# A linear-attention and two-MLP kernel: attention units of two head pairs by two chunks in six equal stages

## The chip, the cores and the metric

The kernel runs on one core of a Trainium2 chip. The metric is the device time of one execution in microseconds. The kernel before took 366.56 us (median of 3 runs, 365.85 to 368.96).

## What is computed

The reference, cut to what matters (batch 2, 8 heads, 768 steps, head size 48, model size 384, hidden size 1024, all float32):

```python
for t in range(S):                      # attention with a decaying state
    cur = np.einsum('bhd,bhe->bhde', u[None] * kt, vt)
    y[:, :, t] = np.einsum('bhd,bhde->bhe', rt, state + cur)
    state = wt[:, :, :, None] * state + np.einsum('bhd,bhe->bhde', kt, vt)
...
xk = mu_k * x + (1.0 - mu_k) * x_prev   # first MLP, x_prev is x one step back
xr = mu_r * x + (1.0 - mu_r) * x_prev
k = np.maximum(xk @ w_k, 0.0)
v = k * k @ w_v
r = 1.0 / (1.0 + np.exp(-(xr @ w_r)))
x = r * v
...
h = gelu(x @ w_in)                      # second MLP, u and v are h's halves
v_s = np.einsum('ts,bsd->btd', w_sg, layernorm(v)) + b_sg[None, :, None]
out = x + (u * v_s) @ w_out
```

## The kernel before

The 12 chunks of 128 steps (6 in each batch) are grouped into five **stages** of 2, 2, 2, 3 and 3 chunks (`CHUNKS`). In a stage there are four attention **units**, one for each pair of heads (`PAIRS`); a head takes 64 of the 128 partitions (`SLOT`), 48 of them used. There are 20 units. A unit passes over the engines in three steps:

- VectorE, `scan` and `scale_keys` (L987 to L1026): running products of the decays w (`prod`), r times k (`rkp`), reciprocals of the ends, `r_in`, the products from the back (`suffix`), and the scaled keys `k_in`.
- TensorE, `first` (L592): coefficients r·k·u into `pkt`, transposes of `k_in`, and the scores into `ps`. ScalarE copies coefficients and transposed keys (`coef`, `k_tok`) and writes the diagonal tiles of `att` (L860), one 128x128 instruction for each chunk and head. VectorE overwrites the part above the diagonal with the scores (`mask`, L1033). TensorE, `second` (L618): keys times values into `pu`. VectorE adds the state (`carry_on`, tile `z`) and ScalarE multiplies it by the decay (L879, tiles `inner` and `carry`).
- TensorE, `third` (L635): state times `r_in` and `att` times values into `py`. ScalarE copies `py` to `y_sb`; SyncE moves it into `X`, from head rows to model rows, with two or three small transfers a unit (`segments`, `give_output`, L463).

Once all four units of a stage are in `X`, ScalarE and VectorE mix it with itself one step back (`xf`) and split it into a high and a low float32r part (`xkr_h`, `xkr_l`). TensorE then computes the **first MLP** of the stage with three matmuls for each product (`three`, L332 to L334: high·high, high·low, low·high): 27 matmuls for r, 72 for k and 72 for v, each as wide as the stage has steps (256 or 384). They are cut into tiles of at most 512 columns in three PSUM banks. ScalarE and VectorE split the squared relu of each k tile again (`k2_h`, `k2_l`, in the trace `k_h`, `k_l`), and v's matmuls wait for it.

The order is set by slots: in slot `i` each engine works unit `i` (VectorE's scan), unit `i - 1` (`first`, `mask`, `second`) and unit `i - 2` (`third`), and the pieces of the first MLP that `PIECES` puts there, from slot `FIRST_MLP` = 7 on. Weights are split into high and low parts in fixed slots (`WSPLIT`). A second, plain form of the attention exists for decays far from 1: ScalarE checks all of w ahead, in four pieces (`flat_w`, L776 and L778), TensorE sums the counts, and at slot `CHOICE` VectorE and SyncE load the flag and branch over the plain form.

SyncE issues every load: `wb` (decays by stage), `rk` and `vb` (by unit), `flat_w`, and the weights.

The **second MLP** (`ORDER2`, 686 of the 2389 matmul records) follows when all stages are done, over all eight PSUM banks.

## Time and profile before

| | |
|---|---|
| median of 3 runs | 366.56 us |
| the profiled execution | 368.12 us, of which the span is 366.4 us |
| TensorE matmuls busy | 333.6 us, 91% of the span |
| VectorE busy | 220.3 us, 60% |
| ScalarE busy | 180.6 us, 49% |
| GpSimd busy | 43.4 us, 12% |
| DMA | 28.98 MB |

The profile is of one execution. Busy time of TensorE is the union of overlapping matmuls with modelled ends. In a timeline "us" is the length of one instruction or of a run of like ones, while the rate is read from one start to the next. A number in brackets is the idle time of the engine just before the instruction, with what ended it. A float32 matmul shows as two records, so "x8" of scores are four matmuls; a float32r matmul (L332 to L334) is one.

### The profile page before, as it was taken

To read this page: it belongs to the slowest core of one execution; us is meant where nothing else is said; L and a number is where in the kernel's file an instruction comes from. 1 tells how busy PE (TensorE), PEld (TensorE's weight loads), DVE (VectorE), ACT (ScalarE), POOL (GpSimd) and SP (SyncE) were. 2 spreads that over 40 slices of the span, in tenths; PEclk is the share of its full clock that TensorE was granted. 3 is DMA by queue.
4 is the path that set the end of the run, shared out by engine and by line. 5 is a ranking of instruction groups with operands and counts; after the bars stand their busy time and mean duration, and the time that the engine had idled before them with its cause. 6 is when DMAs were issued, how large, how long until landed. Compare 5 with 4: busy or idle time off the path is not lost.

```text
span 366.4 us, 6535 instructions
## 1 busy us (share of the span) xinstructions
PE 333.6 (91%) x2389; PEld 311.6 (85%) x2389; DVE 220.3 (60%) x417; ACT 180.6 (49%) x404; POOL 43.4 (12%) x54
## 2 busy tenths in 40 slices
PE   3876649969999899979999999999999999999996
PEld 2654439968899789968999999989999998999996
DVE  5567672896489866788448548369363445503332
ACT  1899565673457565756558457256511303521110
POOL 2000000000000000000000000027423303803320
PEclk9999958989999989998999999999999999999999
DMA  7997114202540242110000601520000030000012
GB/s 212 401 362 231 55 53 143 56 5 69 174 136 13 83 118 62 51 40 16 18 16 2 226 7 24 237 86 0 2 0 2 0 108 23 1 2 0 2 43 86
DMA packets 15632, 28.98 MB, mean 79 GB/s; under 512 B 2160, under 2 KB 10224, under 8 KB 15600
## 3 DMA queue, kind: packets, MB, share of 16 engines
q1 hardware_dynamic: 15600, 28.56, 23.7%
q8 instruction: 19, 0.31, 0.4%
q14 instruction: 13, 0.11, 0.1%
HBM read 23.83 MB, written 2.36 MB: 71 GB/s over the span
## 4 chain that ended last, share of the span: by engine, by line
PE 69%; DVE 13%; ACT 9%; issue 7%; DMA 1%; DVEq 1%; SPq 0%; ACTq 0%
PE pm L332 14%; PE pm L334 13%; PE pm L333 13%; PE ps L334 3%; PE ps L333 3%; PE ps L332 3%; DVE att L1033 2%; ACT att L860 2%; PE py L649 2%; PE ps L614 2%; PE py L655 2%; DVE suffix L1014 2%; DVE prod L996 1%; DVE xf L1076 1%; PE pkt L334 1%
## 5 line engine op out<-in xcount | busy, mean ns | idle before, releaser
L332 PE MATMUL pm<-k_h,wv_h 128*128 128x256 f32 (+1 forms) x120 | 38.4, 320 | 2.8 <-issue 2.8
L556 POOL TENSOR_TENSOR rstd<-vare,half_neg 128x1 f32<-128x1 f32 x12 | 9.4, 784 | 261.0 <-DVE vare L1186 261.0
L334 PE MATMUL pm<-k_h,wv_l 128*128 128x256 f32 (+1 forms) x120 | 37.5, 313 | 0.0
L333 PE MATMUL pm<-k_l,wv_h 128*128 128x256 f32 (+1 forms) x120 | 37.5, 312 | 0.0
L332 PE MATMUL pm<-xkr_h,wk_h 128*128 128x256 f32 (+1 forms) x120 | 37.3, 311 | 0.0
L334 PE MATMUL pm<-xkr_h,wk_l 128*128 128x256 f32 (+1 forms) x120 | 36.4, 304 | 0.0
L333 PE MATMUL pm<-xkr_l,wk_h 128*128 128x256 f32 (+1 forms) x120 | 36.4, 303 | 0.0
L1100 DVE TENSOR_TENSOR sq<-relu 128x384 f32<-128x384 f32 (+1 forms) x28 | 17.2, 614 | 28.6 <-ACT relu L813 28.4
L860 ACT ACTIVATE att<-ident,coef 128x128 f32<-128x128 f32 x96 | 30.3, 394 | 0.0
L935 ACT CAST gated_h<-gf 128x384 fp32r<-128x384 f32 x16 | 8.2, 514 | 42.9 <-DVE gf L1208 42.9
L879 ACT ACTIVATE inner<-z,prod 128x128 f32<-128x128 f32 x28 | 11.2, 402 | 34.1 <-DVE z L1053 22.1
L332 PEld LDWEIGHTS pm<-k_h,wv_h 128*128 128x128 f32 x120 | 24.0, 200 | 4.2 <-issue 4.2
L614 PE MATMUL ps<-r_in,k_in 48*128 48x128 f32 x192 | 19.7, 339 | 8.0 <-DVE att L1033 8.0
L614 PEld LDWEIGHTS ps<-r_in,k_in 48*128 48x128 f32 x192 | 15.3, 226 | 12.8 <-issue 12.8
L813 ACT ACTIVATE relu<-pm 128x384 f32<-128x384 f32 (+1 forms) x28 | 14.9, 533 | 18.8 <-PE pm L334 18.6
L333 PEld LDWEIGHTS pm<-k_l,wv_h 128*128 128x128 f32 x120 | 24.1, 200 | 0.0
L334 PEld LDWEIGHTS pm<-k_h,wv_l 128*128 128x128 f32 x120 | 23.9, 199 | 0.0
L332 PEld LDWEIGHTS pm<-xkr_h,wk_h 128*128 128x128 f32 x120 | 22.8, 190 | 1.0 <-issue 0.7
L333 PEld LDWEIGHTS pm<-xkr_l,wk_h 128*128 128x128 f32 x120 | 22.8, 190 | 0.0
L334 PEld LDWEIGHTS pm<-xkr_h,wk_l 128*128 128x128 f32 x120 | 22.8, 190 | 0.0
L601 PE MATMUL pkt<-par,rkp 128*128 128x2 f32 x96 | 16.0, 277 | 6.4 <-DVE rkp L1001 6.4
L583 POOL TENSOR_TENSOR gated_l<-gf,gated_h 128x384 fp32r<-128x384 f32 x16 | 16.2, 1011 | 46.7 <-ACT gated_h L935 36.5
(227 smaller groups left out, 915.3 us busy)
## 6 DMA issues: line engine op xcount, KB each, us to landing
rk<-in_rkT SPq DMA_DIRECT2D x12, 256.0 KB, 3.8
rk<-in_rkT SPq DMA_DIRECT2D x8, 384.0 KB, 3.4
flat_w<-in_w SPq DMA_DIRECT2D x4, 576.0 KB, 9.5
wsg_raw<-in_wsgT SPq DMA_DIRECT2D x1, 2304.0 KB, 10.4
out_y<-y_out SPq DMA_DIRECT2D x12, 192.0 KB, 1.9
wb<-in_wT SPq DMA_DIRECT2D x2, 776.0 KB, 4.8
vb<-in_vT SPq DMA_DIRECT2D x12, 128.0 KB, 3.6
wk_raw<-in_moe_w_k SPq DMA_DIRECT2D x3, 512.0 KB, 11.2
```

The source lines that it names most:

```text
L332: pe.matmul(o, a_h, b_h, start=first and n == 0, stop=False)
L333: pe.matmul(o, a_h, b_l, start=False, stop=False)
L334: mm = pe.matmul(o, a_l, b_h, start=False, stop=last and n == len(pairs) - 1)
L556: pool.tensor_tensor(rstd[:, t:t + 1], vare[:, t:t + 1], half_neg[:], ALU.pow).then_inc(rstd_done, 1)
L583: pool.tensor_tensor(gated_l[:, x, cols], gf[:, ng % 2], gated_h[:, x, cols], ALU.subtract).then_inc(gl_done, 1)
L601: pe.matmul(pkt[:, MAXT + 2 * ch:MAXT + 2 * ch + 2], rkp[:, p, ch * C:(ch + 1) * C], u_col[:, g], start=True, stop=True)
L614: mm = pe.matmul(ps[:, h, cols], k_in[head, p, cols], r_in[head, un % 3, cols], start=True, stop=True)
L813: act.activation(relu[:, j % 2, 0:G * T], o, ACT.Relu).then_inc(m_free[bk], 1)
L860: last = act.activation(att[:, b % 2, h, ch * C:(ch + 1) * C], ident[:], ACT.Identity, scale=coef[:, b % 2, 2 * ch + h:2 * ch + h + 1])
L879: act.activation(to, z[:, zi % NZ], ACT.Identity, scale=prod[:, b % 2, ch, C:C + 1]).then_inc(state_done, 1)
L935: act.copy(gated_h[:, x, cols], gf[:, ng % 2]).then_inc(gh_done, 1)
L1100: dve.tensor_tensor(sq[:, j % 2, both], relu[:, j % 2, both], relu[:, j % 2, both], ALU.mult).then_inc(sq_done, 1)
```

## The change

- All stages have two chunks (`N` = 2), so there are six, each with two units; a unit holds two head pairs by two chunks, four blocks of 128 steps (`BLOCKS`). There are 12 units. In stage `s`, the loops below call the next stage's units `a` = 2s + 2 and `b` = 2s + 3.
- The inputs of a unit (decays, r, k) come in one load of 790 KB (`load_unit`); for unit 0 it is split, the decays on SyncE's queue and r and k on ScalarE's, which also loads the parameters.
- Coefficients go to the end of `pu`, beside the key-value products, so `first` waits for the state steps of the unit before (`z_done`). The state keeps 64 columns for a head pair; TensorE reads only the 48 rows of a head. VectorE does all state steps, four 128x128 ones for both pairs of a unit, and ScalarE none.
- The check of w is done by unit, on the loaded decays, and the choice is made for each stage; the plain form, if chosen, runs for that stage.
- All first-MLP tiles are 256 wide. The orders of SyncE, TensorE, ScalarE and VectorE are written out, with loops over the stages.
- `mixed`, `gf` and `vf` of the second MLP have other places in memory. The second MLP's instructions and their order are the same.

```diff
-CHUNKS = ((0, 0, 2), (0, 2, 2), (0, 4, 2), (1, 0, 3), (1, 3, 3))
-LONGEST = 3
 PAIRS = 4
+N = 2
+T = N * C
+BLOCKS = 2 * N
+WIDE = BLOCKS * C
+W1 = BLOCKS * (C + 1) + 1
+UNIT = W1 + 2 * WIDE
...
+            def load_unit(un):
+                if un == 0:
+                    sp.dma_start(inw[:, 0, 0:W1], units[:, 0:W1]).then_inc(s_in[0], 16)
+                    return
+                if un >= 3:
+                    sp.wait_ge(kin_done, un - 2)
+                    sp.wait_ge(rkp_done, un - 2)
+                    sp.wait_ge(checked, un - 2)
+                sp.dma_start(inw[:, un % 3], units[:, un * UNIT:(un + 1) * UNIT]).then_inc(s_in[un % 3], 16)
...
+            def give_output(un):
+                s, q, _, _ = place(un)
+                sp.wait_ge(y_done, un + 1)
+                for pr in range(2):
+                    for row, kt, f, m in segments(2 * q + pr):
+                        sp.dma_start(X[f:f + m, s % 2, kt, 1:T + 1],
+                                     y_sb[row:row + m, un % 2, pr * T:(pr + 1) * T]).then_inc(x_in[q], 16)
...
+            load_unit(0)
+            load_unit(1)
+            load_v(0)
+            load_part(0)
+            load_v(1)
+            load_part(1)
+            load_part(2)
+            load_unit(2)
+            load_part(3)
+            load_v(2)
+            for j in parts_of("wv"):
+                load_part(j)
+            give_output(0)
+            give_output(1)
+            choose(0)
+            for s in range(STAGES - 1):
+                for un in (2 * s + 3, 2 * s + 4):
+                    if un < NU:
+                        load_unit(un)
+                        load_v(un)
+                give_output(2 * s + 2)
+                give_output(2 * s + 3)
+                choose(s + 1)
...
                 if un:
                     pe.wait_ge(coef_done, un)
+                    pe.wait_ge(z_done, z_count(un))
+                for m in range(BLOCKS):
+                    mm = pe.matmul(pu[:, COEF + 2 * m:COEF + 2 * m + 2], rkp[:, p, m * C:(m + 1) * C],
+                                   u_col[:, 2 * q + m // N], start=True, stop=True)
+                if q == 1:
+                    pe.wait_ge(checked, un + 1)
+                    mm = pe.matmul(pu[0:1, FLAG:FLAG + un + 1], ones[:], outside[:, 0:un + 1], start=True, stop=True)
+                mm.then_inc(c_mm, 1)
+                pe.wait_ge(kin_done, un + 1)
+                if un:
...
+                pe.wait_ge(inner_done, un + 1)
+                if c0:
+                    pe.wait_ge(carry_done, carry_count(un - 1))
...
+                pe.wait_ge(att_done, un + 1)
...
-            for i in range(SLOTS):
-                b, c = unit(i, 1), unit(i, 2)
-                before, after = parts(i)
-                if b is not None:
+            first(0)
+            second(0)
+            first(1)
+            second(1)
+            third(0)
+            third(1)
+            for s in range(STAGES):
+                a, b = 2 * s + 2, 2 * s + 3
+                if 0 < s < STAGES - 1:
+                    first(a)
+                    second(a)
+                for tile in RS + KS[:1]:
+                    first_mlp(s, *tile)
+                if s == 0:
+                    first(a)
+                    second(a)
+                    for tile in KS[1:]:
+                        first_mlp(s, *tile)
+                    third(a)
                     first(b)
-                if c is not None:
-                    third(c)
-                for tile in before:
-                    first_mlp(*tile)
-                if b is not None:
                     second(b)
-                for tile in after:
-                    first_mlp(*tile)
-                if i == CHOICE:
-                    pe.wait_ge(outside_done, NCHK)
-                    pe.matmul(pm[0][0:1, 0:NCHK], ones[:, 0:1], outside[:], start=True, stop=True).then_inc(flag_sum, 1)
+                    first_mlp(s, *VS[0])
+                    third(b)
+                    first_mlp(s, *VS[1])
+                else:
+                    if s < STAGES - 1:
+                        third(a)
+                        first(b)
+                        second(b)
+                    for tile in KS[1:]:
+                        first_mlp(s, *tile)
+                    if s < STAGES - 1:
+                        third(b)
+                    for tile in VS:
+                        first_mlp(s, *tile)
...
+            act.dma_start(inw[:, 0, W1:UNIT], units[:, W1:UNIT]).then_inc(s_first, 16)
+            act.dma_start(par[:], params).then_inc(s_par, 16)
...
-            def check(n):
-                act.activation(q, q, ACT.Square, bias=minus_one[:, 0:1]).then_inc(sq_w, 1)
...
+                decays = inw[:, un % 3, 0:W1 - 1].rearrange("p (m t) -> p m t", m=BLOCKS)[:, :, 1:C + 1]
+                act.activation(junk[:], decays, ACT.Square, bias=minus_one[:, 0:1]).then_inc(sq_w, 1)
+                act.wait_ge(sq_w, un + 1)
+                act.activation(junk[:], junk[:], ACT.Relu, bias=minus_one[:, 0:1], scale=RANGE ** -2,
+                               accum_out=outside[:, un:un + 1]).then_inc(checked, 1)
...
-                        to = inner[:, b % 2, ch] if ch < n - 1 else carry[:, g, s % 2]
-                        act.activation(to, z[:, zi % NZ], ACT.Identity,
-                                       scale=prod[:, b % 2, ch, C:C + 1]).then_inc(state_done, 1)
...
+            check(0)
+            act.wait_ge(s_par, 16)
+            coefs(0)
+            keys(0)
+            diagonals(0)
+            check(1)
+            coefs(1)
+            diagonals(1)
+            keys(1)
+            high_weight(0)
+            high_weight(1)
+            output(0)
+            high_weight(2)
+            output(1)
+            high_weight(3)
+            mix(0)
+            for s in range(STAGES):
+                a, b = 2 * s + 2, 2 * s + 3
+                more = s < STAGES - 1
+                if s and more:
+                    coefs(a)
+                    keys(a)
+                    diagonals(a)
+                if more:
+                    check(a)
+                gate(s, *RS[0])
+                gate(s, *RS[1])
+                key_high(s, 0)
+                if more:
+                    check(b)
+                if s == 0:
+                    coefs(a)
+                    keys(a)
+                    diagonals(a)
+                    for n in range(1, KG):
+                        key_high(s, n)
+                        high_weight(parts_of("wv")[n - 1])
+                    high_weight(parts_of("wv")[KG - 1])
+                    output(a)
+                    coefs(b)
+                    keys(b)
+                    diagonals(b)
+                    output(b)
+                    mix(s + 1)
+                elif more:
+                    output(a)
+                    coefs(b)
+                    keys(b)
+                    diagonals(b)
+                    for n in range(1, KG):
+                        key_high(s, n)
+                    output(b)
+                    mix(s + 1)
+                else:
+                    for n in range(1, KG):
+                        high_weight(parts_of("win")[n - 1])
+                        key_high(s, n)
                     split_x2(0)
...
+                added = pu[:, 0:COEF].rearrange("p (r c e) -> p r c e", r=2, c=N)
+
+                def total(ch):
+                    return prod[:, p, ch:BLOCKS:N, C:C + 1].to_broadcast([P, 2, SLOT])
+
                 dve.wait_ge(u_mm, un + 1)
+                if un:
+                    dve.wait_ge(inner_done, un)
+                if c0:
+                    dve.wait_ge(carry_done, carry_count(un - 1))
+                    dve.tensor_tensor(z[:, 0], added[:, :, 0], carry[:, (s - 1) % 2, q], ALU.add).then_inc(z_done, 1)
+                else:
+                    dve.tensor_copy(z[:, 0], added[:, :, 0]).then_inc(z_done, 1)
+                dve.wait_ge(z_done, z_count(un) + 1)
+                if un >= 2:
+                    dve.wait_ge(y_mm, un - 1)
+                dve.tensor_tensor(inner[:, p], z[:, 0], total(0), ALU.mult).then_inc(inner_done, 1)
+                if len(steps(un)) == N:
+                    dve.wait_ge(inner_done, un + 1)
+                    if carry_count(un):
+                        dve.wait_ge(carry_done, carry_count(un))
+                    dve.tensor_tensor(z[:, 1], added[:, :, 1], inner[:, p], ALU.add).then_inc(z_done, 1)
+                    dve.wait_ge(z_done, z_count(un + 1))
+                    dve.tensor_tensor(carry[:, s % 2, q], z[:, 1], total(1), ALU.mult).then_inc(carry_done, 1)
...
+                mix_now(s, 0)
+                mix_now(s, 1)
+                mix_low(s, 0)
+                mix_now(s, 2)
+                mix_low(s, 1)
+                mix_low(s, 2)
...
+            scan(0)
+            scan_back(0)
+            dve.wait_ge(s_par, 16)
+            dve.tensor_scalar(omu[:], mu, -1.0, 1.0, ALU.mult, ALU.add).then_inc(omu_done, 1)
+            scan(1)
+            scan_back(1)
+            mask(0)
+            carry_on(0)
+            mask(1)
+            carry_on(1)
+            low_weight(0)
+            scan(2)
+            choose(0)
+            dve.wait_ge(omu_done, 1)
+            mix(0)
+            for j in parts_of("wk"):
+                low_weight(j)
+            scan_back(2)
+            for s in range(STAGES):
+                a, b = 2 * s + 2, 2 * s + 3
+                if s == 0:
+                    key_low(s, 0)
+                    mask(a)
+                    carry_on(a)
+                    key_low(s, 1)
+                    scan(b)
+                    key_low(s, 2)
+                    scan_back(b)
+                    key_low(s, 3)
+                    for j in parts_of("wv"):
+                        low_weight(j)
                     mask(b)
                     carry_on(b)
-                for tile in after:
-                    first_mlp(*tile)
-                for j in range(len(WSPLIT)):
-                    if WSPLIT[j][4] == i:
-                        low_weight(j)
-                if i == END + 2:
-                    split_x2(0)
-                if i == CHOICE:
-                    choose()
+                    scan(b + 1)
+                    scan_back(b + 1)
+                    choose(s + 1)
+                    mix(s + 1)
+                elif s < STAGES - 1:
+                    mask(a)
+                    carry_on(a)
+                    scan(b)
+                    scan_back(b)
+                    key_low(s, 0)
+                    mask(b)
+                    carry_on(b)
+                    key_low(s, 1)
+                    if b + 1 < NU:
+                        scan(b + 1)
+                    key_low(s, 2)
+                    if b + 1 < NU:
+                        scan_back(b + 1)
+                    key_low(s, 3)
+                    choose(s + 1)
+                    mix(s + 1)
+                else:
+                    key_low(s, 0)
+                    for n in range(1, KG):
+                        low_weight(parts_of("win")[n - 1])
+                        key_low(s, n)
+                    for kt in range(KT):
+                        split_x2(0, kt)
+                for tile in VS:
+                    value(s, *tile)
```

TensorE at the start of the program. Before, units follow one another with `third` (L649, L655) of unit 0 after `first` (L601, L605, L614) of unit 1:

```order
L601 MATMUL pkt<-par,rkp 128x2 x2
L605 MATMUL pkt<-ident,k_in 128x128 x2
L614 MATMUL ps<-r_in,k_in 128x128 x4
L629 MATMUL pu<-vb,k_tok 64x64 x4
L601 MATMUL pkt<-par,rkp 128x2 x2
L605 MATMUL pkt<-ident,k_in 128x128 x2
L614 MATMUL ps<-r_in,k_in 128x128 x4
L649 MATMUL py<-r_in,inner 64x128 x2
L655 MATMUL py<-att,vb 64x128 x4
L629 MATMUL pu<-vb,k_tok 64x64 x4
L601 MATMUL pkt<-par,rkp 128x2 x2
L605 MATMUL pkt<-ident,k_in 128x128 x2
```

All of six such units pass before the first L332. After, with four blocks a unit, from the transposes of unit 0 on (L540, L544, L550 and L559 are `first`, L576 `second`, L598 and L605 `third`):

```order
L550 MATMUL pkt<-ident,k_in 128x128 x4
L559 MATMUL ps<-r_in,k_in 128x128 x8
L576 MATMUL pu<-vb,k_tok 64x64 x8
L540 MATMUL pu<-par,rkp 128x2 x4
L544 MATMUL pu<-outside,ones 1x2
L550 MATMUL pkt<-ident,k_in 128x128 x4
L559 MATMUL ps<-r_in,k_in 128x128 x8
L576 MATMUL pu<-vb,k_tok 64x64 x8
L598 MATMUL py<-r_in,inner 64x128 x4
L605 MATMUL py<-att,vb 64x128 x8
L598 MATMUL py<-r_in,inner 64x128 x4
L605 MATMUL py<-att,vb 64x128 x8
```

The row after the last one is the first matmul of the first MLP. Both `third` have moved behind both `second`, and two units stand before the MLP where six stood.

VectorE in the middle of the program. Before, between the mix of stage 1 and that of its third tile (L1086 is `xkr_l`, L1114 the product with v, L1033 `mask`, L1053 the state, L996 to L1023 the scans):

```order
L1086 TENSOR_TENSOR xkr_l<-xf,xkr_h 128x2x256 x2
L1114 TENSOR_TENSOR x_116<-pm,x_116 128x2x256
L1033 COPY_PREDICATED att<-upper,ps 128x2x256
L1053 TENSOR_TENSOR z<-pu,carry 128x128
L1076 SCALAR_TENSOR_TENSOR xf<-X,omu,xf 128x256 x2
L996 SCALAR_TENSOR_TENSOR prod<-wb,one 128x258
L1001 TENSOR_TENSOR rkp<-rk 128x256
L1005 RECIPROCAL ends<-prod 128x2
L1008 TENSOR_TENSOR r_in<-rk,prod 128x256
L1014 SCALAR_TENSOR_TENSOR suffix<-wb,ends 128x258
L1023 TENSOR_TENSOR k_in<-rk,suffix 128x256
L1086 TENSOR_TENSOR xkr_l<-xf,xkr_h 128x2x256
```

After, between the mix of stage 3 and the first k tile (L1077, L1114, L1030 and L1048 to L1061 are the same steps):

```order
L1114 TENSOR_TENSOR x_116<-pm,x_116 128x256
L1030 COPY_PREDICATED att<-upper,ps 128x1024
L1048 TENSOR_TENSOR z<-pu,carry 128x128
L1054 TENSOR_TENSOR inner<-z,prod 128x128
L1059 TENSOR_TENSOR z<-pu,inner 128x128
L1061 TENSOR_TENSOR carry<-z,prod 128x128
L997 SCALAR_TENSOR_TENSOR prod<-inw,one 128x516
L1003 TENSOR_TENSOR rkp<-inw 128x512
L1007 RECIPROCAL ends<-prod 128x4
L1010 TENSOR_TENSOR r_in<-inw,prod 128x512
L1018 SCALAR_TENSOR_TENSOR suffix<-inw,ends 128x516
L1023 TENSOR_TENSOR k_in<-inw,suffix 128x512
```

The four state operations now stand in a row on VectorE, each waiting for the one before. The scans of the stage's second unit have moved behind mask and states of its first unit, and the whole mix of a stage stands in one piece ahead of them.

## Rows read from the trace of the kernel before

**Rows 1.** Windows by stage of the first MLP: us, busy us of each engine, PEclk.

```profile
core 0: us, PE busy (x) PEld busy (x) DVE busy (x) ACT busy (x) POOL busy (x), PEclk, DMA share, GB/s
0.00:54.50 54.50, 32.59 (x228) 25.37 (x228) 36.32 (x83) 35.99 (x85) 1.92 (x14) 0.91 0.64 218
54.50:93.70 39.20, 35.74 (x318) 32.93 (x316) 26.92 (x57) 23.46 (x58) 0.00 (x0) 0.91 0.26 75
93.70:132.00 38.30, 36.18 (x355) 33.23 (x353) 29.76 (x59) 22.67 (x63) 0.00 (x0) 0.97 0.33 105
...
209.20:238.80 29.60, 29.60 (x172) 29.60 (x172) 16.45 (x25) 14.89 (x25) 0.00 (x0) 1.00 0.29 103
238.80:366.40 127.60, 124.67 (x686) 120.12 (x684) 58.38 (x103) 37.12 (x66) 41.44 (x40) 1.00 0.08 25
```

**Rows 2.** Timeline of TensorE, 256-wide matmuls: start, us, instruction.

```profile
94.13 0.28 PE L332 MATMUL pm<-xkr_h,wr_h 128*128 128x256 f32 x1
...
94.49 0.28 PE L332 MATMUL pm<-xkr_h,wr_h 128*128 128x256 f32 x1
```

**Rows 3.** Timeline of TensorE, attention between MLP matmuls, two and three chunks.

```profile
99.62 0.50 PE L601 MATMUL pkt<-par,rkp 128*128 128x2 f32 x4
...
102.00 0.39 PE L332 MATMUL pm<-xkr_h,wk_h 128*128 128x256 f32 x1
...
181.64 0.72 PE L601 MATMUL pkt<-par,rkp 128*128 128x2 f32 x6
...
185.01 0.44 PE L332 MATMUL pm<-xkr_h,wk_h 128*128 128x384 f32 x1
```

**Rows 4.** Timeline of VectorE: front halves of a two-chunk and a three-chunk unit, masks.

```profile
92.61 0.70 DVE L996 TENSOR_TENSOR_SCAN prod<-wb,one 128x258 f32<-128x258 f32 x1 [0.58 <-ACT inner L879]
...
95.00 0.74 DVE L1033 COPY_PREDICATED att<-upper,ps 128x512 f32<-128x512 uint32 x1
...
122.76 0.96 DVE L996 TENSOR_TENSOR_SCAN prod<-wb,one 128x387 f32<-128x387 f32 x1
...
126.08 0.69 DVE L1086 TENSOR_TENSOR xkr_l<-xf,xkr_h 128x512 fp32r<-128x512 f32 x1
...
127.02 1.00 DVE L1033 COPY_PREDICATED att<-upper,ps 128x768 f32<-128x768 uint32 x1
```

**Rows 5.** The page: GB/s moved in 40 equal slices of 9.16 us.

```profile
GB/s 212 401 362 231 55 53 143 56 5 69 174 136 13 83 118 62 51 40 16 18 16 2 226 7 24 237 86 0 2 0 2 0 108 23 1 2 0 2 43 86
```

**Rows 6.** Timeline of TensorE: the same score matmuls early and late.

```profile
37.92 1.23 PE L614 MATMUL ps<-r_in,k_in 48*128 48x128 f32 x8
...
62.81 0.72 PE L614 MATMUL ps<-r_in,k_in 48*128 48x128 f32 x8
```

**Rows 7.** Timelines of ScalarE and SyncE, the chain, DMA issues (us to landing).

```profile
114.43 1.86 ACT L860 ACTIVATE att<-ident,coef 128x128 f32<-128x128 f32 x6
...
23.53 1.80 SPq L463 DMA_DIRECT2D X<-y_sb  x3
...
X<-y_sb SPq DMA_DIRECT2D x22, 48.0 KB, 2.0
...
40.93 0.54 DVEq L979
```

**Rows 8.** Groups by form: engine, operation, count, busy us, mean ns, idle before.

```profile
L1076 DVE SCALAR_TENSOR_TENSOR xf<-X,omu,xf 128x256 f32<-128x256 f32 x18 | 7.7, 481 | 2.7 <-ACT xf L790 2.5
L1086 DVE TENSOR_TENSOR xkr_l<-xf,xkr_h 128x512 fp32r<-128x512 f32 x9 | 5.9, 686 | 0.7 <-ACT xkr_h L799 0.7
L1120 DVE TENSOR_TENSOR wv_l<-wv_raw,wv_h 128x768 fp32r<-128x768 f32 x4 | 3.6, 951 | 0.0
L1100 DVE TENSOR_TENSOR sq<-relu 128x512 f32<-128x512 f32 x12 | 8.3, 690 | 14.7 <-ACT relu L813 14.7
L778 ACT ACTIVATE flat_w<-flat_w,minus_one 128x1152 f32<-128x1152 f32 x4 | 5.0, 1255 | 0.1
```

**Rows 9.** Timeline of TensorE at a wait, and the window around it.

```profile
161.97 0.94 PE L614 MATMUL ps<-r_in,k_in 48*128 48x128 f32 x12 [2.11 <-DVE att L1033]
...
159.00:170.00 11.00, 8.82 (x82) 7.91 (x82) 9.52 (x17) 5.18 (x14) 0.00 (x0) 0.84 0.16 45
```

880 lines of the change are left out of this document (347 added, 533 removed).

## The prediction

> **What bounds the kernel now.** I began with the busy shares on the page: TensorE 91% of the span, VectorE 60%, ScalarE 49%. The reader should see there that TensorE looks like the bound, and distrust it, since its ends are modelled and an average hides stages. So next comes the table by stage [rows 1], cut where the first MLP's matmuls of each stage begin. The span falls into three parts. From 0 to 54.5 the first MLP has not started; TensorE is busy 32.6 of 54.5 us with small matmuls. From 54.5 to 238.8 the five stages run; the first two take 39.2 and 38.3 us, the last 29.6. From 238.8 to 366.4 the second MLP runs, 127.6 us, at full clock and busy nearly throughout. The diff leaves the third part's instructions and their order alone, so I take it as unchanged and forecast only when it starts.
>
> Matmul rates come from start to start, not from the "us" column: a 256-wide matmul follows the one before it after 0.12 us (0.36 for three) [rows 2], a 384-wide one after 0.173 (171 of them fill the last stage, 29.6 us) [rows 1]. An attention unit of two chunks takes 2.38 us from its coefficients to the end of its outputs, one of three chunks 3.37 [rows 3].
>
> **The matmul work.** Before, the first MLP is 3 stages of 171 at 0.12 and 2 of 171 at 0.173: 61.3 + 59.3 = 120.6 us. After, it is 6 x 171 x 0.12 = 122.6, so 2 us more. Per column a narrow matmul is dearer than its width: 256 columns at 2.4 GHz are 0.107 us and 384 are 0.16, both 0.013 below the rows. The Trainium skill ("TensorE: Matmul & The Clock Gate", section "Wait — 56ns, not 53.3ns?") puts the fixed part at about 2.5 ns for one matmul; by it the sixth stage's 171 extra matmuls would cost 0.4 us. By the rows they cost 2, and I use the rows. Attention: four blocks, extrapolated from 2.38 and 3.37, take 4.4, and their key-value products about 0.6: 5.0 us a unit, 10 a stage. A full stage is then 20.4 + 10.0 + 0.5 of changeovers = 31 us of TensorE. The work is the same as before; the term that can change is what TensorE waits for.
>
> **The start.** Before, four units of stage 0 (and two more) have to pass before any MLP. After, two fat units do. Chain, in us from the span's start. VectorE works a unit's front half (products, reciprocals, r_in, suffix, k_in) in 2.39 for two chunks and 3.32 for three [rows 4], so 4.25 for four blocks. The data of unit 0 are 0.8 MB: at 212 GB/s in the first slice [rows 5] 3.7 us after issues near 1, and a first latency near 1: in at about 5.8, and its keys ready at 9.4. TensorE is slow here: eight score matmuls' records take 1.23 us at 37.9 and 0.72 at 62.8 [rows 6], while the granted clock is given as 0.91 on average [rows 1]; the two durations are those of its two levels, 1.2 and 2.4 GHz, so I price its work until the MLP at 1.7 times. Transposes 1.2, key copy 0.6, eight diagonals at 0.295 (1.86 for six [rows 7]) end at 13.9; the mask (0.74 for 512, 1.00 for 768 elements [rows 4], so 1.27 for 1024) and two state steps end at 16.1. `first(1)` now waits for those (z_done, a new wait: behind it on TensorE stand unit 1's coefficients, transposes and scores and both `third`, and ScalarE's `coefs(1)` waits for them), then 1.3 + 1.2 + 2.3 and `second(1)` 1.3: 22.4. `third(0)` and `third(1)` at 3.0 each: 28.4. Output copy 0.6. Then SyncE issues five X transfers a unit at 0.6 each (1.80 for three [rows 7]); the last lands 2.0 after its issue [rows 7]: 33.6. The mix of stage 0 (two 0.48 steps, a cast and a 0.69 subtraction for each of three kt [rows 8], ScalarE in between) takes 4.7 after that. First MLP matmul at 38 instead of 54.5: **16 us early**.
>
> Unit 0's second half comes on ScalarE's queue. The Trainium skill ("Trainium Kernel Development and Optimization", section "Key Constraints") says that transfers issued from SP and ACT share the same 16 DMA engines and interleave, so the extra queue saves issue time only. By it unit 1's 790 KB share the engines with unit 0's 524 KB; the 5.8 above would be 6.5 and the start 0.7 later. No run here shows two queues.
>
> **Stage 0** gives much of that back. First stage: slow clock over its first 3.4 us (1.7 lost, as at 54.5); `second(2)` waits for the keys behind ScalarE's checks (1.1); `first(3)` waits for VectorE's suffix scan behind two key subtractions (2.3); the v tiles wait for the four wv subtractions (0.95 each [rows 8]), which VectorE reaches after `key_low(0, 3)` (2.5). Worst is the end: `third(3)` stands between the two v tiles, so its output, 4.5 us of transfers and 4.7 of mixing have 2.9 us of v matmuls and 2.5 of `first(4)` as cover. That leaves TensorE waiting 5 to 7 us, and the r matmuls of stage 1 start at about 85. Stage 0 lasts 46.5 us against 39.2: **7.3 lost**.
>
> **Stages 1 to 4.** VectorE's work in one: two front halves 8.5, masks 2.5, states 3.0 (eight operations of about 0.28 and a hand-over), four key pairs 5.6 (2 x 0.69 each [rows 8]), mix 4.4, v products 1.0, `choose` 1.1 (its load of the flag 0.54 [rows 7] and the branch): 26. Below 31, but it is not free to slide. The chain from the end of one stage's v tiles: coefficients and transposes 1.4, keys 0.65, diagonals 2.45, mask 1.3, states 1.5, front half of b 4.35: 11.65. `key_low(0)` 1.4, then a wait for b's diagonals until 15.4, mask and states 18.2, key pair 19.6, scan 22.05, key pair 23.45, suffix 25.35, last key pair 26.75. TensorE stands at the last quarter of v's first sum at 24.65 and so waits 2.1 us; 6.45 us of v matmuls follow. Period **33.2**, against 31 for TensorE alone. A wait of 2.1 us is in the trace once [rows 9], and TensorE's clock is low after it (0.84 in 159 to 170); 3.3 us of matmuls at half rate cost 1.65. I count that in about half of the stages. Stage 1 is 1.5 shorter (last chunks have no second state). Stage 4 has no scans ahead and no wait, so 31; its mix ends 1 us late.
>
> Sum: r matmuls of stage 1 at 85; v ends 31.7, 33.2, 33.2 and 30.5 later counted from 82.5, which gives 211; mix wait 1.4; last stage 20.4 and 1.2 behind the w_in subtractions: 234. Half of four slow spells would add 3, and against it I take off 2 for handovers counted twice: the second MLP starts at **235 instead of 238.8**. Span 362.6, with the 1.7 around it 364.3 against the profiled 368.1. The runs' median is 366.56, so I forecast 366.6 - 4 = **362.5**.
>
> **Bounds of what no row shows.** A four-block step lies between the three-chunk row and twice the two-chunk row: front half 3.3 to 4.8, mask 1.0 to 1.5, attention unit 3.4 to 4.8; I take the continued line from two to three. A state step with a broadcast factor lies between 0.28 and 0.35 and a hand-over of 0.1 comes on top. `choose` costs VectorE 0.5 to 1.1. Each of these at its upper end lengthens a stage's chain by 1 to 1.5 us, at its lower end shortens it by the whole 2.1.
>
> **Edits that I price at nothing.** The check of w moves from four 1152-wide pairs on ScalarE to twelve 512-wide ones (10 us becomes about 15) and 2.3 MB of loads go. One 1152-wide step is 1.25 [rows 8]; by width and a fixed part a 512-wide one is about 0.65. ScalarE is at 23 busy of 38 in a stage [rows 1]. If the cover fails (a check stands before `coefs(a)` in stage 0) it is 1.4 each, 5 in all. State decays leave ScalarE (40 operations) for 22 small ones on VectorE, in the chain above. X transfers: 50 before, 60 after, since each stage has ten. On SyncE's queue they now stand behind the next two units' loads, whose waits (`kin_done`, `y_mm` of the stage before) are over by then, so nothing is added; were one of them late, X and with it the mix would be late by the same. The 48 state rows for 128 change no column count; between nothing and 0.1 us a unit.
>
> **Rivals.**
> (B) VectorE keeps up. If b's diagonals come earlier or the state steps are shorter, the waits disappear and so do the slow spells: 3 x 2.1, 1.4 and 1.2 less than 234, and the same 2 off: second MLP at 223, 16 earlier, time **351**. For it: VectorE has 26 of 31. Against: the chain crosses four engines and I found no slack in it.
> (C) The other side. The chain is the bound in every stage and grows with hand-overs of 0.1 to 0.2 that I left out. It decides from a period of 35.5 on: 2.3 more in four stages and 1.65 of slow clock in two more, 235 + 9.2 + 3.3 = 247.5, which is 8.7 after 238.8: **375**. For it: before, the stages lose 4 to 7 us to such waits already, and their loose order (one unit behind) gives more slack than the new one.
> (D) The start is not early. Two-chunk units of two pairs double every latency of the chain; if unit 0's data land at 8 and the X transfers queue behind the wv loads, the MLP starts at 43, five later than forecast: second MLP at 240, time **368**. For it: half of the chain is slow TensorE. Against: 6.9 MB are in by 22 us at the rates of the first slices (212, 401 and 362 GB/s) [rows 5], before X is needed.
>
> **How the numbers follow.** Forecast 0.45 (its own range 358 to 367), B 0.22, C 0.20, D 0.13. A measurement here can tell about 1%, 3.7 us. Faster than 362.9: 0.6 of the forecast's share and B's, 0.48. Within 1%: 0.31. Slower: most of C and a little of D, 0.21. The range leaves out the far halves of B and C: 353 to 374.
>
> **What would show it.** Right: first MLP matmul near 38; its wait for v tiles and X around 70 to 84; stages 1 to 3 of 33 to 35 us; a 2 us wait of TensorE on k_l in the first v tile of each, with a fall of its clock after; the second MLP starting near 235 and lasting 127.6. Wrong: stage periods of 31 (B) or over 35.5 (C), a start after 42 (D), or a second MLP whose length differs, which I have no reason for.

## The result, and the profile after

The changed kernel takes 369.6 us (median of 6 runs, 368.3 to 371.1) against 366.8 (6 runs of the kernel before): ratio 1.008, 95% interval 1.004 to 1.011. That is within 1%, on the slow side. The forecast was 362.5, faster.

The profiled execution took 370.85 us, with a span of 369.1. These are the windows of the changed kernel, cut where each stage's first MLP matmuls begin, so that they answer to [rows 1]:

```profile
core 0: us, PE busy (x) PEld busy (x) DVE busy (x) ACT busy (x) POOL busy (x), PEclk, DMA share, GB/s
0.00:38.50 38.50, 18.14 (x139) 15.17 (x139) 21.62 (x39) 20.56 (x46) 2.15 (x14) 1.00 0.62 224
38.50:88.10 49.60, 41.37 (x361) 38.72 (x361) 32.05 (x50) 24.66 (x58) 0.00 (x0) 0.87 0.18 62
88.10:122.40 34.30, 33.36 (x320) 31.44 (x317) 23.41 (x40) 20.81 (x51) 0.00 (x0) 0.94 0.25 83
122.40:157.00 34.60, 32.45 (x313) 30.51 (x309) 24.11 (x42) 20.24 (x50) 0.00 (x0) 0.95 0.22 74
157.00:190.00 33.00, 31.62 (x322) 29.69 (x318) 24.02 (x42) 20.19 (x50) 0.00 (x0) 1.00 0.15 45
190.00:219.30 29.30, 28.38 (x275) 26.82 (x274) 18.03 (x31) 18.67 (x45) 0.00 (x0) 1.00 0.16 45
219.30:241.50 22.20, 20.72 (x171) 20.55 (x172) 12.86 (x17) 12.07 (x17) 0.00 (x0) 1.00 0.41 157
241.50:369.10 127.60, 124.69 (x687) 120.09 (x685) 58.25 (x103) 37.13 (x66) 41.49 (x40) 1.00 0.07 25
```

The first MLP starts at 38.5 instead of 54.5 and the second lasts the same 127.6. Yet the second starts at 241.6 instead of 238.8. In the 38.5 us before the first MLP TensorE is idle for 38.5 - 18.1 = 20.4; in the 54.5 of before it was 54.5 - 32.6 = 21.9 [rows 1]. So the early start saves 1.5 us of idle time. The other 14.5 are busy time: 228 matmul records stood ahead of it before, 139 do now, and the difference, which is attention work, comes behind it. Next, the six longest of TensorE's nine waits over 0 to 242 us (us in total, times, longest):

```profile
PE pm L292 <- DVE xkr_l L1077: 10.6, 2, 9.6
PE pu L540 <- DMA par<-in_params: 7.5, 1, 7.5
PE pu L576 <- ACT k_tok L758: 6.1, 3, 4.9
PE pm L292 <- DVE k_l L1105: 5.7, 4, 1.9
PE pu L540 <- DVE z L1059: 2.3, 1, 2.3
PE pkt L550 <- DVE k_in L1023: 1.5, 1, 1.5
```

The forecast has each of them, except that it has the first one as a wait for unit 0's data and keys and not for the parameters (`par`). What it did not price stands in the timeline of TensorE in stage 0:

```profile
60.38 0.19 PE L544 MATMUL pu<-outside,ones 128*1 128x4 f32 x2
62.03 1.12 PE L550 MATMUL pkt<-ident,k_in 128*128 128x128 f32 x4 [1.46 <-DVE k_in L1023]
63.08 2.08 PE L559 MATMUL ps<-r_in,k_in 48*128 48x128 f32 x16
65.08 1.12 PE L576 MATMUL pu<-vb,k_tok 128*64 128x64 f32 x16
67.06 0.55 PE L292 MATMUL pm<-k_h,wv_h 128*128 128x256 f32 x1 [0.85 <-issue]
67.41 0.41 PE L293 MATMUL pm<-k_l,wv_h 128*128 128x256 f32 x1
67.62 0.41 PE L294 MATMUL pm<-k_h,wv_l 128*128 128x256 f32 x1
```

Behind a wait of 1.46 us the scores take 2.08 us (1.16 at the fast level), and the v matmuls follow every 0.21 us instead of every 0.12 [rows 2]. The windows show the granted clock there, and in two more stretches:

```profile
64.00:70.00 6.00, 5.14 (x42) 4.76 (x40) 5.90 (x10) 2.12 (x8) 0.00 (x0) 0.50 0.03 9
...
88.00:92.00 4.00, 4.00 (x22) 3.88 (x21) 2.69 (x6) 3.25 (x10) 0.00 (x0) 0.50 0.21 83
147.00:151.00 4.00, 4.00 (x24) 4.00 (x23) 3.74 (x8) 3.18 (x7) 0.00 (x0) 0.60 0.94 329
```

0.50 is 1.2 GHz of 2.4; the last window also holds 0.8 us at full clock. The stretch at 88 follows the long wait at the end of stage 0, the one at 147 follows a wait of 1.93 us for `k_l`. The end of stage 0 stands in the timelines of ScalarE (first three rows) and TensorE:

```profile
77.18 0.59 ACT L775 COPY y_sb<-py 128x512 f32<-128x512 f32 x1 [11.06 <-PE py L605]
77.67 0.91 ACT L785 ACTIVATE xf<-X,par 128x256 f32<-128x256 f32 x2
83.32 0.91 ACT L785 ACTIVATE xf<-X,par 128x256 f32<-128x256 f32 x2 [4.75 <-issue]
...
81.42 1.16 PE L559 MATMUL ps<-r_in,k_in 48*128 48x128 f32 x16
87.52 0.69 PE L576 MATMUL pu<-vb,k_tok 128*64 128x64 f32 x8 [4.94 <-ACT k_tok L758]
```

The outputs of unit 3 end at 77.1, their X transfers and the mix at 87.6. TensorE has the second v tile and unit 4's first half as cover, and then waits 4.94 us.

### The profile page after: what moved, and what is told of

Same layout as the page of the kernel before. It is cut to its first block, busy times and chain, and to the rows that moved or that the text cites. A ratio compares the mean times of both kernels' runs of the same rounds, so it can differ in the third digit from the quotient of the medians.

```text
span 369.1 us, 6660 instructions
## 1 busy us (share of the span) xinstructions
PE 330.7 (90%) x2570; PEld 313.0 (85%) x2570; DVE 214.4 (58%) x361; ACT 174.3 (47%) x377; POOL 43.6 (12%) x54
## 4 chain that ended last, share of the span: by engine, by line
PE 67%; DVE 14%; issue 9%; ACT 7%; DMA 2%; SPq 1%; DVEq 0%; ACTq 0%
PE pm L292 12%; PE pm L293 11%; PE pm L294 11%; ACT att L766 3%; PE ps L293 3%; PE ps L294 3%; PE ps L292 3%; DVE sq L1100 2%; PE py L605 2%; DVE prod L997 2%; PE py L598 2%; DVE suffix L1018 2%; PE pu L540 2%; PE ps L559 2%; PE py L293 1%
## 5 line engine op out<-in xcount | busy, mean ns | idle before, releaser
L292 PE MATMUL pm<-k_h,wv_h 128*128 128x256 f32 x144 | 43.3, 301 | 6.6 <-DVE k_l L1105 5.7
L293 PE MATMUL pm<-k_l,wv_h 128*128 128x256 f32 x144 | 42.4, 294 | 0.0
L294 PE MATMUL pm<-k_h,wv_l 128*128 128x256 f32 x144 | 42.3, 294 | 0.0
L292 PE MATMUL pm<-xkr_h,wk_h 128*128 128x256 f32 x144 | 41.3, 287 | 0.0
L293 PE MATMUL pm<-xkr_l,wk_h 128*128 128x256 f32 x144 | 40.7, 283 | 0.0
L294 PE MATMUL pm<-xkr_h,wk_l 128*128 128x256 f32 x144 | 40.7, 283 | 0.0
L292 PEld LDWEIGHTS pm<-k_h,wv_h 128*128 128x128 f32 x144 | 29.3, 203 | 8.3 <-issue 8.3
L1030 DVE COPY_PREDICATED att<-upper,ps 128x1024 f32<-128x1024 uint32 x12 | 16.3, 1354 | 33.4 <-ACT att L766 28.4
L293 PEld LDWEIGHTS pm<-k_l,wv_h 128*128 128x128 f32 x144 | 29.3, 204 | 0.0
L294 PEld LDWEIGHTS pm<-k_h,wv_l 128*128 128x128 f32 x144 | 29.3, 204 | 0.0
L785 ACT ACTIVATE xf<-X,par 128x256 f32<-128x256 f32 x36 | 16.4, 504 | 24.1 <-issue 12.0
L292 PE MATMUL pm<-xkr_h,wr_h 128*128 128x256 f32 x54 | 18.0, 333 | 10.6 <-DVE xkr_l L1077 10.6
L817 ACT ACTIVATE relu<-pm 128x512 f32<-128x512 f32 x24 | 14.4, 598 | 22.8 <-PE pm L294 21.9
L1100 DVE TENSOR_TENSOR sq<-relu 128x512 f32<-128x512 f32 x24 | 16.5, 686 | 10.6 <-ACT relu L817 10.6
L540 PE MATMUL pu<-par,rkp 128*128 128x2 f32 x96 | 13.7, 264 | 9.8 <-DMA par<-in_params 7.5
```

The lines of the kernel that those rows point to most:

```text
L292: pe.matmul(o, a_h, b_h, start=first and n == 0, stop=False)
L293: pe.matmul(o, a_h, b_l, start=False, stop=False)
L294: mm = pe.matmul(o, a_l, b_h, start=False, stop=last and n == len(pairs) - 1)
L540: mm = pe.matmul(pu[:, COEF + 2 * m:COEF + 2 * m + 2], rkp[:, p, m * C:(m + 1) * C], u_col[:, 2 * q + m // N], start=True, stop=True)
L785: act.activation(xf[:, kt, n], X[:, s % 2, kt, 1:T + 1], ACT.Identity, scale=mu[:, n, kt:kt + 1]).then_inc(t_done, 1)
L817: act.activation(relu[:, j % 2], pm[bk][:], ACT.Relu).then_inc(m_free[bk], 1)
```

## The experiments

"Starts" are those of the six stages' first MLP matmuls and then of the second MLP, from TensorE's timeline. Ratios are to the kernel before, run beside each.

| kernel | median us | ratio, 95% interval | starts, us |
|---|---|---|---|
| before | 366.8 | 1 | 54.5, 93.7, 132.0, 173.1, 209.2, then 238.8 |
| changed | 369.6 | 1.008 (1.004 to 1.011) | 38.5, 88.1, 122.4, 157.0, 190.0, 219.3, then 241.6 |
| before_six_stages | 371.9 | 1.013 (1.011 to 1.015) | 54.6, 93.6, 127.1, 160.9, 194.3, 221.7, then 242.6 |
| third_early | 364.3 | 0.994 (0.992 to 0.995) | 38.6, 84.2, 116.7, 149.8, 182.7, 212.0, then 234.3 |
| weights_early | 364.2 | 0.993 (0.991 to 0.995) | 38.5, 81.9, 115.7, 150.2, 183.1, 212.3, then 234.6 |
| scans_late | 363.0 | 0.990 (0.988 to 0.992) | 38.0, 86.8, 119.4, 150.4, 181.9, 211.1, then 233.4 |
| no_decay_check | 367.6 | 1.002 (1.001 to 1.004) | 38.7, 86.2, 120.5, 154.8, 187.7, 217.0, then 239.3 |
| x_two_queues | 374.2 | 1.022 (1.018 to 1.025) | 37.3, 85.5, 122.7, 158.0, 193.0, 222.8, then 245.0 |
| three_moves | 356.9 | 0.973 (0.971 to 0.975) | 38.6, 82.1, 113.4, 144.4, 175.7, 204.9, then 227.2 |
| key_between | 351.9 | 0.960 (0.957 to 0.963) | 38.0, 77.7, 109.0, 139.9, 171.3, 200.5, then 222.8 |
| spin_fitted | 349.4 | 0.954 (0.950 to 0.959) | 35.6, 72.1, 103.4, 134.4, 165.7, 196.0, then 218.3 |

**The sixth stage and the narrow matmuls alone.**

```diff
-CHUNKS = ((0, 0, 2), (0, 2, 2), (0, 4, 2), (1, 0, 3), (1, 3, 3))
+CHUNKS = ((0, 0, 2), (0, 2, 2), (0, 4, 2), (1, 0, 2), (1, 2, 2), (1, 4, 2))
```

> The kernel before with its two stages of three chunks replaced by three of two, all else as it was (units of one head pair, the old order, the checks as they were for this table of chunks). It measures the price of narrower matmuls and of a sixth stage by themselves. Theory W (by the rows: a 256-wide matmul 0.12 us, a 384-wide 0.173): 171 x (6 x 0.12 - 3 x 0.12 - 2 x 0.173) = 2.3 us more matmul time, and one more changeover with its waits of TensorE, 2 to 5 us as in its other stages: 371 to 374. Rival N (the page's 2.5 ns of fixed cost a matmul, and TensorE's waits hidden as before): 0.4 us more, 367. Rival P (the three-chunk stages were the badly balanced ones, since VectorE and ScalarE have longer work there): 366 or less.

Theory W: 371.9, and the stages last 188.0 us instead of 184.3. Its windows:

```profile
160.90:194.30 33.40, 32.70 (x318) 29.95 (x316) 24.58 (x56) 19.50 (x55) 0.00 (x0) 1.00 0.15 42
194.30:221.70 27.40, 25.38 (x228) 24.00 (x226) 14.09 (x27) 13.54 (x32) 0.00 (x0) 1.00 0.12 31
221.70:242.60 20.90, 20.75 (x171) 20.58 (x172) 12.61 (x16) 12.16 (x17) 0.00 (x0) 1.00 0.49 183
```

A pure stage of 171 narrow matmuls lasts 20.9 us, 0.122 each, against 29.6 for 171 wide ones [rows 1]. The six stages alone cost 4.8 us against the runs of the kernel before beside them (367.1). The rest of the change (fat units, early start, written order) gives about 2 of them back; its parts were not separated.

**The end of stage 0.** The outputs of unit 3 ahead of both v tiles:

```diff
-                    first_mlp(s, *VS[0])
                     third(b)
-                    first_mlp(s, *VS[1])
+                    for tile in VS:
+                        first_mlp(s, *tile)
```

> The changed kernel with the outputs of unit 3 put ahead of both v tiles of stage 0 instead of between them; nothing else moves. Theory T (the end of stage 0 is the chain outputs of unit 3, y_sb copy, ten X transfers, mix): in the changed kernel that chain runs from 77.07 (end of the outputs) to 88.14. With the outputs first they wait for VectorE's state steps (69.3) and end at 71.3; the chain then ends at 82.3, while TensorE's v tiles and unit 4's first half end near 81.5. Stage 1 starts 5 to 6 us earlier (82 to 83 instead of 88.1), the time falls to 364 to 365. Rival S (it is TensorE's low clock that costs, and a new wait of 2 us for the states at 67 slows the v tiles for longer): the v tiles run at half rate, stage 1 starts at 85 or later and the time is 367 or more. Rival M (the middle stages are bound by their own chain on ScalarE and VectorE, which gives the time back): stage 1 starts early but stages 1 to 3 grow from 34.3, 34.6 and 33.0, and the second MLP still starts at 240 or later.

Theory T, except that stage 1 starts at 84.2 and not at 82 to 83. Against the changed kernel 5.3 us of median are gone. Two rows of its TensorE timeline, and then three windows:

```profile
61.46 0.66 PE L550 MATMUL pkt<-ident,k_in 128*128 128x128 f32 x4 [1.46 <-DVE k_in L1023]
...
68.03 0.69 PE L598 MATMUL py<-r_in,carry 48*64 48x128 f32 x4 [4.20 <-DVE inner L1054]
```

```profile
38.60:84.20 45.60, 38.97 (x361) 36.54 (x361) 32.48 (x51) 24.99 (x58) 0.00 (x0) 0.93 0.21 75
84.20:116.70 32.50, 31.57 (x321) 29.66 (x317) 22.87 (x38) 20.52 (x51) 0.00 (x0) 1.00 0.25 78
116.70:149.80 33.10, 30.96 (x313) 29.00 (x309) 24.02 (x42) 20.20 (x50) 0.00 (x0) 1.00 0.23 78
```

The same wait of 1.46 us is followed here by fast transposes (0.66). Now TensorE waits 4.20 us for the states, then works 5.7 us at half rate (68.0 to 73.7). But the idle time ahead of stage 1 is gone, and stage 1 runs at full clock. Stages 1 and 2 are 1.8 and 1.5 us shorter with not one instruction of them changed: the slow stretches at 88 and at 147 are gone. The second of them is gone although the wait for `k_l` ahead of it is as long as before:

```profile
140.21 0.35 PE L292 MATMUL pm<-k_h,wv_h 128*128 128x256 f32 x1 [1.92 <-DVE k_l L1105]
```

**VectorE's load in stage 0.** Casts and subtractions of wk and wv moved into the idle time around the first mix, unit 3's scans ahead of the first key pair (VectorE's part; ScalarE's casts of wv move likewise):

```diff
-            mix(0)
-            for j in parts_of("wk"):
+            for j in parts_of("wk")[:2]:
+                low_weight(j)
+            mix(0, parts_of("wk")[2:] + parts_of("wv")[:1])
+            for j in parts_of("wv")[1:]:
                 low_weight(j)
             scan_back(2)
+            scan(3)
+            scan_back(3)
...
-                    key_low(s, 1)
-                    scan(b)
-                    key_low(s, 2)
-                    scan_back(b)
-                    key_low(s, 3)
-                    for j in parts_of("wv"):
-                        low_weight(j)
+                    for n in range(1, KG):
+                        key_low(s, n)
```

> The changed kernel with the casts and subtractions of the wk and wv weights moved into the idle time of ScalarE and VectorE around the first mix (22 to 42 us), and unit 3's scans moved ahead of stage 0's first key pair; third still between the v tiles. In the changed kernel the wv subtractions take VectorE 63.3 to 66.8, and unit 3's k_in comes at 62.0, for which TensorE waits 1.46 us and then runs the scores and half of the first v tile at half clock. Theory C (that wait and its fall of clock cost 1.5 + about 3 us, all of which passes to the end of stage 0, since the chain behind unit 3's outputs moves with them): stage 1 starts at 83 to 84.5 instead of 88.1, time 365 to 366. Rival K (the clock falls anyway, from the other waits of stage 0, or the tail takes all of it): stage 1 at 87 or later, time 368.5 or more. In both, the first MLP starts at 38 to 40.

Theory C. The wait for `k_in` is gone, the scores of unit 3 take 1.16 us and the first v tile follows at 62.60 at 0.12 a matmul; stage 1 starts 6.2 us earlier than in the changed kernel, at 81.9, 1 below what was expected. The edit takes away two things at once, the late `k_in` and the wv subtractions ahead of the v tile: that tile starts 4.5 us earlier (67.06 before), and its full rate is worth 1.9 more. Whether the fall of clock in the changed kernel was an accident of one execution was asked of a second profile:

> The changed kernel once more, unaltered, for a second profile. In its first profile TensorE's granted clock was low from 62 to 71.5 us behind a wait of 1.46 us; with the outputs of unit 3 ahead of the v tiles, the same wait at 60 us was followed by matmuls at full rate. Theory F (the fall is a property of this order of work): it is there again between 62 and 72, and stage 0 lasts 49 to 50 us. Rival V (whether the clock falls behind a wait of 1 to 2 us varies from execution to execution): the low stretch is absent or elsewhere, stage 0 lasts 47 to 48, and the spell of the first profile is not to be charged to the change.

Theory F: the starts are the same within 0.2 us, and the window from 64 to 70 again reads 0.50. So the spell comes back with this kernel. It does not follow from TensorE's order of work alone: `x_two_queues` (below) has the same order there and the same wait, and no fall behind it. TensorE's timeline there, and the wv subtractions on VectorE, first in the changed kernel and then in `x_two_queues`:

```profile
60.44 0.66 PE L559 MATMUL pkt<-ident,k_in 128*128 128x128 f32 x4 [1.46 <-DVE k_in L1033]
61.02 1.16 PE L568 MATMUL ps<-r_in,k_in 48*128 48x128 f32 x16
...
65.46 0.36 PE L292 MATMUL pm<-k_h,wv_h 128*128 128x256 f32 x1 [2.67 <-issue]
...
63.29 3.56 DVE L1120 TENSOR_TENSOR wv_l<-wv_raw,wv_h 128x768 fp32r<-128x768 f32 x4
...
61.69 3.56 DVE L1130 TENSOR_TENSOR wv_l<-wv_raw,wv_h 128x768 fp32r<-128x768 f32 x4
```

In both kernels the v tile starts 0.2 us behind the end of these subtractions (66.85 and 65.25), whether the scores before it took 2.08 us (a wait of 0.85) or 1.16 (a wait of 2.67). So the 1.8 us that the slow transposes, scores and state products took longer were hidden behind VectorE. What was passed on is the loss in the v tile itself: 20 matmuls at half rate, 1.9 us, and 17 with 1.6 us in `x_two_queues`. `scans_late`, whose stage 0 is the changed kernel's, agrees: a wait of 0.41 for `k_in`, scores of 1.16, and 2.67 ahead of the v tile.

**The waits of the middle stages.** The scans for the next stage behind the last key pair:

```diff
-                    key_low(s, 1)
+                    for n in range(1, KG):
+                        key_low(s, n)
                     if b + 1 < NU:
                         scan(b + 1)
-                    key_low(s, 2)
-                    if b + 1 < NU:
                         scan_back(b + 1)
-                    key_low(s, 3)
```

> The changed kernel with the scans of the next stage's first unit (scan and scan_back, 4.3 us of VectorE) moved in stages 1 to 3 from between the key pairs to behind the last of them. Theory B (TensorE's waits of 0.94, 1.93 and 1.38 us in the first v tile are VectorE's, and only because these scans stand in front of the last subtraction): the last k_l comes 1.9 to 4 us earlier, all three waits go (4.2 us), and with them the spells of half clock of stages 1 and 2 (1 to 2 us each): stages 1 to 3 of 32.5 to 33, time 363 to 365. Rival R (the last key pair is bound by ScalarE's relu and square, which stand behind diagonals(b)): the waits stay above 0.5 us each and the time is within 1 us of 369.6. Rival L (the scans are now late for the next stage's transposes or hold up the mix): a new wait of TensorE on k_in or xkr_l of over 1 us in each stage, time 369 or more.

Theory B, and more: 363.0. TensorE's waits on `k_l` from stage 1 on were 5.7 us in four; now the row is

```profile
PE pm L292 <- DVE k_l L1105: 1.5, 1, 1.5
```

which is the one of the last stage. Stages 1 to 3 last 32.6, 31.0 and 31.5 us. That is 6.8 us less: 4.2 of waits, 1.6 of the slow spell at 147 (the window from 140 to 152 now reads 1.00), and 1 us that is not resolved. That the spell went because of the wait is not shown: in `third_early` it was absent with the wait in place. The start and stage 0, where nothing was changed, are 0.5 and 0.8 us shorter in this profile; the medians differ by 6.6.

**ScalarE's checks.** The kernel leaves out the check of the decays, and takes the flag as zero.

```diff
-                act.activation(junk[:], decays, ACT.Square, bias=minus_one[:, 0:1]).then_inc(sq_w, 1)
-                act.wait_ge(sq_w, un + 1)
-                act.activation(junk[:], junk[:], ACT.Relu, bias=minus_one[:, 0:1], scale=RANGE ** -2,
-                               accum_out=outside[:, un:un + 1]).then_inc(checked, 1)
+                act.activation(outside[:, un:un + 1], minus_one[:], ACT.Relu).then_inc(checked, 1)
```

> The changed kernel without the check of the decays: each unit's two 512-wide operations on ScalarE (1.65 us with their read of the sum) become one of a single column, and the flag is always zero; its product with ones on TensorE, its copy and the choice on VectorE and SyncE stay. Theory A (ScalarE is the late engine of the chain: the check of unit b stands ahead of coefs(b) and its diagonals, for which VectorE waits 28.4 us in all, and VectorE is late for the last key pair because of it): the waits of TensorE on k_l in stages 1 to 3 (0.94, 1.93 and 1.38 us) vanish with their spells of low clock, stages 1 to 3 last 32 us, k_tok in stage 0 comes 1 us earlier, time 363 to 365. Rival O (the checks lie in ScalarE's idle time, and VectorE is bound by its own scans between the key pairs): the waits stay within 0.3 us, time 368 to 369.

Rival O, 0.4 below its range: 367.6, and the waits on `k_l` stay at 5.7 us. The 2.0 us come from stage 0 (47.5 us instead of 49.6), where one check stands ahead of `coefs(a)`; TensorE's wait of 0.98 us for `k_tok` there is gone. In the middle stages VectorE's mask waits as long as before, since the diagonals wait for TensorE's coefficients and not for ScalarE:

```profile
100.43 1.37 DVE L1026 COPY_PREDICATED att<-upper,ps 128x1024 f32<-128x1024 uint32 x1 [4.60 <-ACT att L762]
```

**The X transfers on two queues**, the second head pair's from ScalarE:

```diff
                 act.copy(y_sb[:, un % 2], py[:]).then_inc(y_done, 1)
+                give_second(act, un)
```

> The changed kernel with each unit's second head pair's X transfers (two or three of five) issued by ScalarE right behind its copy of the outputs, the other half by SyncE as before. Theory Q (the X transfers are bound by the 0.59 us that SyncE takes to issue each): the ten take 3 to 3.5 us instead of 6.85 from the first issue to the last; the first MLP starts 2 to 2.5 us earlier (36 instead of 38.5), the wait at the end of stage 0 shrinks by as much or 2.5 more, since there all ten count: stage 1 at 83 to 85 instead of 88.1, time 365. Rival E (the transfers share the same DMA engines, so that only issue time is saved and their landings stretch): start 38, stage 1 at 87.5, time 369. Rival A (issuing costs ScalarE 0.6 us each too, and pushes back its casts and the copies of the keys): 370 to 373.

Theory Q for the start (37.3, 1.2 us earlier, half of what it expected) and rival A for the rest, beyond its range: 374.2. In stage 1, ScalarE's timeline:

```profile
96.44 2.10 ACTq L361 DMA_DIRECT2D X<-y_sb  x3
98.64 0.17 ACT L758 COPY coef<-pu 128x8 f32<-128x8 f32 x1 [2.23 <-issue]
```

Three issues hold ScalarE 2.23 us ahead of b's coefficients and transposed keys. In stages 1 to 4 TensorE now waits 1.4 to 1.7 us each for `k_tok`, 6.2 in all, which it did not before, and these stages are 6.1 us longer; nothing there waits for X. The split of units 0 and 1 alone came later:

> The kernel with three moves, and the X transfers of units 0 and 1 alone shared between SyncE's and ScalarE's queues. With all units shared the first MLP began at 37.3 instead of 38.5, but stages 1 to 3 lengthened by 2.9, 0.7 and 2.0 us. Theory Q2 (ScalarE's 0.6 us an issue did that, in stages where its chain is the late one; at the start it is idle): start at 37.3, stages 0 to 4 as in three moves, time 355.5 to 356. Rival D2 (with the wv casts now in this idle time, ScalarE has no room, and they are 1 us later): start at 38.3 or later, time 356.5 or more.

Rival D2: 357.3 against 356.9, start at 39.3. With the weights' casts in that idle time, ScalarE has no room for the issues: they hold it for 2.23 and 1.48 us ahead of two of these casts.

**The three together.**

> The changed kernel with all three: outputs of unit 3 ahead of stage 0's v tiles, weights and unit 3's scans early, scans late in stages 1 to 3. In profiles the first two gave 7.3 and 6.9 us alone. Theory I (they share the tail of stage 0: with VectorE free at 63 its mask and states come at 65.5 to 67, so that the outputs end at 69 and the chain behind them at 80): stage 1 starts at 79.5 to 80.5, then TensorE's own work of about 31.5 a stage, 28.9 and 22.3: the second MLP at 225 to 228, time 356 to 359. Rival J (the two remove the same loss, and without TensorE's waits to hide it the first half of the next unit is what is left): stage 1 at 82, second MLP at 230 or later, time 360 to 362.

The start of stage 1 is rival J's (82.1), the end is theory I's: second MLP at 227.2, 356.9 us. Two windows:

```profile
82.10:113.40 31.30, 31.30 (x320) 29.58 (x318) 23.03 (x38) 20.38 (x51) 0.00 (x0) 1.00 0.22 72
113.40:144.40 31.00, 30.78 (x312) 28.99 (x310) 24.02 (x42) 20.12 (x50) 0.00 (x0) 1.00 0.27 92
```

TensorE is busy throughout: these are the 31 us of "TensorE alone" in the forecast. What was left in stage 0 was a wait of 3.13 us for unit 3's state, so its last key tile went there (TensorE's part of the edit):

```diff
-                    for tile in KS[1:]:
+                    for tile in KS[1:3]:
                         first_mlp(s, *tile)
                     third(a)
                     first(b)
                     second(b)
+                    first_mlp(s, *KS[3])
                     third(b)
```

> The kernel with three moves, and in stage 0 the last key tile put between unit 3's state products and its outputs (ScalarE's and VectorE's parts of that tile behind b's diagonals and states), as the other stages have it. In the profile of three moves TensorE waits there 3.13 us for VectorE's state (62.8 to 65.93) and then works 3.5 us at half rate. Theory H (the key tile's 2.15 us cover the wait and the fall of clock goes with it): stage 0 shrinks by 3 to 5 us (second MLP at 222.5 to 224.5 instead of 227.2), time 352 to 354. Rival X (the outputs of unit 3 end only 2 us earlier, and behind them ten X transfers and the mix then end the stage, since the v tiles that cover them are no longer): stage 1 starts at 80.5 or later, time 355.5 or more.

Theory H: the wait is 0.85 us, stage 1 starts at 77.7, 351.9 us.

**The slow level of the start.** Matmuls of the identity by itself, read by nobody, in TensorE's idle stretches; 28 before the first unit, 16 before the second, 56 before the first MLP:

```diff
+            def spin(n):
+                for _ in range(n):
+                    pe.matmul(pm[0][:, 0:P], ident[:], ident[:], start=True, stop=True)
+
+            spin(28)
             pe.wait_ge(s_par, 16)
```

> The kernel with three moves, and with matmuls of the identity by itself, whose results nobody reads, in TensorE's idle stretches of the start: 28 before the first unit, 16 before the second, 56 between the last outputs and the first MLP. In every profile the small matmuls before 29 us take 1.7 times as long as later (16 score matmuls 2.08 us against 1.16), though the granted clock is shown as 1.00. Theory Z (TensorE's slow level there is due to its idleness before, and extra matmuls lift it): the scores take 1.16 us from the first or second unit on, the first MLP starts 2 to 4 us earlier and its first matmuls follow every 0.12 us from the start; second MLP at 222 to 225 instead of 227.2, time 352 to 355. Rival Y (the level of the start is fixed by time or by the chip and not by what TensorE does): the durations before 29 us stay, and the spare matmuls, at half rate, stand in the way: start at 38.6 or later, time 356 to 360.

> Key tile between, warm start and shared X transfers of units 0 and 1 together, and unit 0's outputs put ahead of unit 1's state products. Theory S (the gains are of different stretches: the key tile 3 to 5 us in stage 0, the others before the first MLP): the first MLP starts at 33 to 35.5 if the start's matmuls can be made fast, 36.5 to 37.5 if not; second MLP at 218 to 221, or 222 to 224; time 347.5 to 351, or 351.5 to 354. Rival U (an earlier start only meets the weights, whose last subtractions end at 41: TensorE waits for wk_l or wv_l instead): start early, but stage 0 longer by as much, time within 1 us of the kernel with the key tile alone.

Both overshot: one such product is two records and takes 0.24 us at the fast level. Still, TensorE's timeline of the first shows the level lifted:

```profile
2.87 9.04 PE L532 MATMUL pm<-ident 128*128 128x128 f32 x56 [2.87 <-POOL upper L489]
...
13.13 1.16 PE L565 MATMUL ps<-r_in,k_in 48*128 48x128 f32 x16
```

1.16 us for unit 0's scores, which take 2.08 in the kernels without them. But the products ahead of unit 0 ran 4 us too long, and the first MLP began at 43.9 (`warm_start`, 359.3 us) and 39.6 (`all_moves`, 349.8: in theory S's range for the time, though the start it rested on, 33 to 35.5, did not come). So two more, with 13 at first; the second has all X transfers on SyncE's queue:

> The kernel with all moves, with 13 identity products ahead of the first unit instead of 28. Each is two matmul records, which I had counted as one: the 28 took 8.64 us and TensorE began the first unit at 11.35 instead of 7.6. Everything behind hangs on that unit. Theory Z2 (the start's chain is shorter by what the slow level had cost, 2 to 3 us, which the overshoot hid): the first unit begins at 7.5 to 8, its 16 scores still take 1.16 us, the first MLP starts at 35.5 to 36.5, second MLP at 218.5 to 219.5, time 345.5 to 347. Rival Y2 (13 are too few to lift the level: scores at 2.08 us again): the start is at 37.5 to 38.5, time 348.5 or more. Rival U2 (the casts and subtractions of the weights then end the start): start early, but TensorE waits for wk_l or wv_l behind it, time 348 or more.

> The same with all X transfers on SyncE's queue. In the kernel with all moves ScalarE was held up 3.28 and 1.48 us by issuing its half of them, ahead of two wk casts. Theory O1 (those holds cost more than the shorter issue time gives, now that the casts stand behind them): 0.5 to 1.5 us faster than the kernel with both queues. Rival O2 (ten issues of 0.59 us on one queue are the longer chain): 1 to 2.5 us slower than with both queues.

351.1 and 350.2, starts at 38.5 and 38.6: the mix ended at 36.1 and 35.3, but the 56 products ahead of it held TensorE. Neither theory is decided by the times. O1 is, by the mix (0.8 us earlier with one queue). Then with 43 of them, and with none before the MLP:

> The kernel with the short spin and one queue, with 43 identity products instead of 56 ahead of the first MLP. In its profile the mix ended at 35.3, but the 56 took until 38.6 (0.24 us each), so that the first MLP still began at 38.6. Theory Z3 (nothing else holds the start): 43 end at 34.9, the first MLP starts at 35.3 to 35.6, its matmuls follow every 0.12 us; second MLP at 217.5 to 218.5 instead of 220.9, time 346.5 to 348. Rival W3 (the weights' subtractions, which end at 38, hold stage 0 then): time 349.5 or more.

> The same with no identity products ahead of the first MLP; those of the first 16 us stay. TensorE idles from 24.5 to 35.3. Theory L3 (the first MLP's matmuls then run at half rate for 3 to 6 us, as they did in the changed kernel, and lose half of that): 1.5 to 3 us slower than the fitted spin, 348.5 to 350. Rival N3 (the first matmuls are then slow, but stage 0 has room for it in its waits for keys and states): within 0.7 us of the fitted spin.

```profile
10.06 1.16 PE L565 MATMUL ps<-r_in,k_in 48*128 48x128 f32 x16
...
24.50 9.87 PE L532 MATMUL pm<-ident 128*128 128x128 f32 x86
35.65 0.36 PE L292 MATMUL pm<-xkr_h,wr_h 128*128 128x256 f32 x1 [1.28 <-ACT wv_h L741]
35.84 0.28 PE L293 MATMUL pm<-xkr_l,wr_h 128*128 128x256 f32 x1
```

With the fitted spin the MLP starts at 35.6 and at the fast level, the second MLP at 218.3. Z3 holds for the profile; the median of 349.4 is above its range, and its runs spread from 348.4 to 351.4, the profiled one being the lowest. Without the last spin the first MLP starts at 36.5 and runs at half rate for some 6 us:

```profile
36.50:42.00 5.50, 5.47 (x26) 5.50 (x26) 5.46 (x7) 3.21 (x5) 0.00 (x0) 0.50 0.13 48
```

Stage 0 then lasts 39.1 us instead of 36.4. The medians, 350.1 and 349.4, do not tell L3 from N3. The slow level of the start is worth about 2.5 us of time between `key_between` (351.9) and `spin_fitted`; how much of that is the level and how much unit 0's outputs ahead of unit 1's state products, which came in the same kernels, was not separated.

The best kernels of the study take 349.4 to 350.2 us, 4.5 to 4.7% less than the kernel before.

## Why the prediction was wrong

- **The start (38): right**, 38.5, and step by step: keys of unit 0 at 9.3 (forecast 9.4), its diagonals at 13.5 (13.9), the last outputs at 28.9 (28.4), the end of the mix at 38.3. The slow level is there too, with scores of 2.08 us against 1.16. In the kernels with spare matmuls and unit 0's outputs moved ahead the mix ends at 35.3; how much of the 3 us is the level was not separated.
- **Matmul price: right.** 0.12 to 0.122 a matmul; the sixth stage alone costs 3.7 us of stages, where the forecast had 2 as matmuls and 0.5 for a changeover. "TensorE: Matmul & The Clock Gate", section "Wait — 56ns, not 53.3ns?", of the Trainium skill has 2.5 ns as the fixed part; the trace disagrees for these matmuls, 0.12 to 0.122 us for 256 columns being 13 to 15 ns above their 0.107.
- **Stage 0 (46.5): the step that failed first**, 49.6, and stage 1 starts at 88.1 instead of 85. Its waits were if anything too dear: 0.98 (forecast 1.1), 1.46 for unit 3's keys (2.3), 0.85 for the wv subtractions (2.5; it was 2.67 behind fast scores in `x_two_queues`), and 4.94 at the end (5 to 7). The missing term is the slow clock. The forecast charged it at the start alone, with 1.7; that was 27 matmuls at 0.213 instead of 0.12, 2.5. It had nothing for the first v tile, where 20 matmuls at half rate lost 1.9, all of it passed to the end of the stage, since unit 3's outputs and X stand behind that tile. Together that is 2.7 us above the forecast, with 3.1 to explain; the smaller waits and the dearer attention work roughly cancel and were not resolved one by one. What brings the clock down at that place is not shown: it was low in the v tile of the changed kernel, `x_two_queues` and `scans_late`, from different moments on.
- **Stages 1 to 4 (31.7, 33.2, 33.2 and, counted from start to start, 29.4): the mechanism right, the sizes off.** They last 34.3, 34.6, 33.0 and 29.3. The waits on `k_l` that the forecast put at 2.1 are 0.94, 1.93 and 1.38. Against that stand two slow spells: 1.8 us in stage 1, behind the wait of 4.94, which the forecast had foreseen as a wait and not as a loss in the stage behind it, and 1.6 at 147. The forecast counted "half of four slow spells", 3 us, so in sum these were right. "Stage 1 is 1.5 shorter" was not: without waits (`three_moves`) it lasts 31.3 us and stage 2 31.0.
- **The last stage (21.6)** lasts 22.3.
- **The 2 us "taken off for handovers counted twice": wrong.** It rested on no row. The steps gave 234, the spells made it 237, and only this subtraction gave 235. Without it the forecast would have been within 1% of the kernel before. The second MLP started at 241.6, 6.6 later than forecast: 3.1 of stage 0, 2 of this subtraction, 0.7 of stages 1 to 4 and 0.7 of the last.
- **The checks: half right.** They cost 2.0 us, not nothing, in the place named (stage 0, ahead of `coefs(a)`), where one takes 1.46 (1.4).
- **Rival C** (the chain is the bound and VectorE late) described stages 1 and 2 (34.3 and 34.6), but its point of decision, a period of 35.5, was not reached. **Rival B** (VectorE keeps up, second MLP at 223, 351 us) has the numbers of `key_between`, 222.8 and 351.9, in part by luck: there stage 0 lasts 39.7 us, after a change of its order that B did not have, and stages 1 to 3 last 31.3, 31.0 and 31.3.
- **The range** (353 to 374) held the time.

The largest error of reading is in none of the terms. "16 us early" was set down as a gain and then spent. Of it 14.5 us were work that TensorE had to do later in any case, and the balance to draw up was TensorE's idle and slow time: up to the second MLP, idle time rose from 29.8 to 35.5 us, and busy time fell from 209.0 to 206.0.

## What to carry to other kernels

An earlier start of the main work is worth the idle time that it removes, not its distance: draw up idle and slow time of the bounding engine before and after. Price each wait of TensorE with the half-rate stretch that may follow it, in the next stage too, and look for what the in-order engine it waits for does just before: moving 4.3 us of work that nobody was waiting for out from between needed steps gained 6.6 us (part of it a slow stretch that may have gone by itself). Subtract nothing that has no row.

## What the runs showed that was not expected

- A wait of 1.46 us was followed by half clock in the changed kernel, in two profiles of two, and by full clock in `third_early` and `x_two_queues`, whose TensorE had done the same work until then. The wait of 1.93 in stage 2 was followed by a slow stretch, the same wait of 1.92 in `third_early` by none; after 0.94 and 1.38 there was none. Neither the length of a wait nor TensorE's order of work tells by itself, and what does is open.
- From 0 to 38.5 and on to 44 us the windows of the changed kernel read a granted clock of 1.00 while matmuls run at the slow rate (2.08 us for 16 records of scores, and 27 MLP matmuls at 0.213 us from 38.5 on). In `key_between`, whose first MLP matmuls follow every 0.213 us as well, the row reads 0.50 from 30 to 38 us. Durations tell the level there, the clock row of the changed kernel does not. The Trainium skill ("TensorE: Matmul & The Clock Gate", section "What's actually happening") has the throttled clock as the default that activity lifts; the spare matmuls agree, with 1.16 us for unit 0's scores.
- A small transfer issued by ScalarE holds it for 0.64 us (median of 30), as it holds SyncE for 0.59 (median of 60, in the changed kernel). Three ahead of a critical copy cost 2.2 us.
